# Splitting a decay step in two on VectorE, and a new order for the first two units, in a gated linear attention with two feed-forward layers

## What is computed

```python
B, H, S, D = 4, 8, 768, 48
state = zeros((B, H, D, D))
for t in range(S):
    state = alpha[:, :, t, :, None] * state + einsum('bhd,bhe->bhde', k[:, :, t], v[:, :, t])
    y[:, :, t] = einsum('bhd,bhde->bhe', q[:, :, t], state)
x = y.transpose(0, 2, 1, 3).reshape(3072, 384)
h = x @ w_in                                    # 384 -> 2048
x = (maximum(h, 0) + slope * minimum(h, 0)) @ w_out
h = x @ w_in2
g = where(h >= 1, h, where(h <= -1, 0, (h + 1) ** 2 / 4))
out = g @ w_out2
```

## Time and profile before

| | |
|---|---|
| median of 3 runs | 930.47 us |
| the profiled execution | 930.54 us, of which the span from first to last instruction is 928.8 us |
| TensorE busy | 906.5 us (98%) |
| VectorE, ScalarE, GpSimd busy | 449.1, 300.7, 293.2 us |
| mean granted TensorE clock | 0.996 of full |

### The profile page before, as it was taken

One profiled execution on the slowest core, in us unless ns is written; L12 is line 12 of the kernel. 1 busy time (PEld: TensorE's weight loads), 2 busy tenths in 40 slices (PEclk: granted clock), 3 DMA queues, 4 the chain that ended last, 5 costly groups with the idle time before them and its releaser, 6 DMA issues.

```text
span 928.8 us, 14324 instructions
## 1 busy us (share of the span) xinstructions
PE 906.5 (98%) x5774; PEld 761.3 (82%) x5774; DVE 449.1 (48%) x614; ACT 300.7 (32%) x561; POOL 293.2 (32%) x267
## 2 busy tenths in 40 slices
PE   8989989999999999999999999999999999999997
PEld 8888978887887888788888888888888888888886
DVE  6886755555655655555335543333333333333332
ACT  3532323223232332332245443233332332332322
POOL 3422212222222222222234334334343243243232
PEclk9999999999999999999999999999999999999999
DMA  8421211211111111110113200000100100100101
GB/s 283 153 68 50 75 42 39 66 40 40 49 40 39 39 40 41 45 60 1 68 35 97 74 1 1 20 14 1 35 1 1 35 0 1 35 1 1 34 1 35
DMA packets 31986, 39.47 MB, mean 42 GB/s; under 512 B 2096, under 2 KB 25136, under 8 KB 31920
## 3 DMA queue, kind: packets, MB, share of 16 engines
q1 hardware_dynamic: 31920, 38.55, 13.8%
HBM read 33.82 MB, written 4.72 MB: 41 GB/s over the span
## 4 chain that ended last, share of the span: by engine, by line
issue 66%; POOL 30%; PE 3%; ACT 0%; POOLq 0%; ACTq 0%
POOL g_lo L342 27%; POOL x_lo L349 2%; PE h_ps L712 1%; POOL p_last L336 0%; POOLq L174 0%; PE y_ps L717 0%; ACT w_hi L383 0%; PE y_ps L719 0%; PE y_ps L718 0%; PE y_ps L658 0%; PE a_ps L658 0%; PE y_ps L680 0%; PE a_ps L680 0%; PE h_ps L717 0%; ACT g L422 0%
## 5 line engine op out<-in xcount | busy, mean ns | idle before, releaser
L342 POOL TENSOR_TENSOR g_lo<-g,g_hi 128x512 fp32r<-128x512 f32 (+1 forms) x208 | 255.2, 1227 | 588.2 <-ACT g_hi L429 588.1
L422 ACT ACTIVATE g<-h_ps 128x512 f32<-128x512 f32 (+1 forms) x208 | 117.6, 565 | 503.5 <-PE h_ps L719 500.6
L717 PE MATMUL h_ps<-x_lo,w_hi 128*128 128x512 f32 (+1 forms) x624 | 240.8, 386 | 11.8 <-DVE x_lo L556 10.1
L717 PE MATMUL y_ps<-g_lo,w_hi 128*128 128x512 f32 (+1 forms) x624 | 233.7, 374 | 1.6 <-POOL g_lo L342 1.4
L719 PE MATMUL h_ps<-x_hi,w_lo 128*128 128x512 f32 (+1 forms) x624 | 233.9, 375 | 0.0
L718 PE MATMUL h_ps<-x_hi,w_hi 128*128 128x512 f32 (+1 forms) x624 | 233.6, 374 | 0.0
L719 PE MATMUL y_ps<-g_hi,w_lo 128*128 128x512 f32 (+1 forms) x624 | 233.0, 373 | 0.0
L718 PE MATMUL y_ps<-g_hi,w_hi 128*128 128x512 f32 (+1 forms) x624 | 232.9, 373 | 0.0
L569 DVE SCALAR_TENSOR_TENSOR g<-g 128x512 f32<-128x512 f32 x96 | 66.5, 692 | 247.0 <-ACT g L422 247.0
L717 PEld LDWEIGHTS h_ps<-x_lo,w_hi 128*128 128x128 f32 x624 | 117.6, 188 | 36.7 <-DVE x_lo L556 11.8
L717 PEld LDWEIGHTS y_ps<-g_lo,w_hi 128*128 128x128 f32 x624 | 118.0, 189 | 23.8 <-POOL g_lo L342 1.7
(11 more groups left out here) (69 smaller groups left out, 484.9 us busy)
## 6 DMA issues: line engine op xcount, KB each, us to landing
qk_sb<-qk SPq DMA_DIRECT2D x24, 448.0 KB, 4.1
y_all<-w SPq DMA_DIRECT2D x16, 384.0 KB, 7.8
alpha_sb<-decays SPq DMA_DIRECT2D x24, 224.0 KB, 3.1
v_sb<-v SPq DMA_DIRECT2D x24, 192.0 KB, 4.0
y<-y_all SPq DMA_DIRECT2D x18, 256.0 KB, 2.6
qk_sb<-w SPq DMA_DIRECT2D x8, 384.0 KB, 3.2
alpha_sb<-w SPq DMA_DIRECT2D x4, 384.0 KB, 3.1
att<-w SPq DMA_DIRECT2D x4, 384.0 KB, 3.0
```

Of the source, the lines that this page charges most:

```text
L342: nc.gpsimd.tensor_tensor(g_lo[:, s % G_RING, 0:w_], g32[:, s % G32_RING, 0:w_], g_hi[:, s % G_RING, 0:w_].bitcast(F32), ALU.subtract).the ...
L422: nc.scalar.activation(g32[:, s % G32_RING, 0:w_], h_ps[s % 2][:, 0:w_], ACT.Relu, scale=-1.0 if first else 0.5, bias=0.0 if first else 0. ...
L717: nc.tensor.matmul(out_, wh, lo, start=start, stop=False)
```

## The change

The decay becomes two stages. `scan_decays(u)` (the two scans and the reciprocal) stands four steps ahead of the turn, so in the step in which unit u - 1 is turned, behind its `x_lo` and behind that step's activation. `scale_qk(u)` (the two multiplications) stands three steps ahead, before that step's activation. For units 0 and 1 the order changes on four engines, unit 1 gets buffers of its own for the token copies of k and of the outputs (in `inv` and `prod`), the outputs of a fresh unit are made head parity by head parity so that they can begin after the first mask, and the identity products are 20 at first and 3 in between.

```diff
-        for _stage, _lag in (("decay", 5), ("scores", 2), ("mix", 1), ("turn", 0)):
+        for _stage, _lag in (("scan", 4), ("scale", 3), ("scores", 2), ("mix", 1), ("turn", 0)):
-ORDER = ("turn", "scores", "mix", "decay")
-FIRST_PLAN = [("scores", 0), ("scores", 1), ("mix", 0), ("turn", 0), ("mix", 1), ("turn", 1)]
-WARM = 24
-FILL = {("scores", 0): 12, ("scores", 1): 1, ("mix", 0): 1, ("turn", 0): 1, ("mix", 1): 2, ("turn", 1): 2}
+ORDER = ("turn", "scores", "mix", "scale", "scan")
+WARM = 20
+FILL = 3
...
+        def k_tok_of(u):
+            return by_pair(inv[:, 0:PAIRS * ROWS]) if u == 1 else k_tok[:]
+
+        def o_tok_of(u):
+            return prod[:, 0:D_MODEL] if u == 1 else o_tok[:].rearrange("p h d -> p (h d)")
...
             copy_k(0)
             split_w(0)
             split_w(1)
+            copy_k(1)
+            split_w(2)
             copy_outputs(0)
-            copy_k(1)
+            copy_outputs(1)
             turn_hi(0)
-            copy_outputs(1)
-            split_w(2)
             turn_hi(1)
...
+            def scale_qk(u):
+                q, k = (qk_of(u)[0:ROWS, x] for x in range(2))
+                dve.wait_ge(qk_loaded[u % 2], 16 * load_count(u))
                 dve.wait_ge(inv_done, u + 1)
-                dve.wait_ge(qk_loaded[u % 2], 16 * load_count(u))
...
             mask(0)
             mask(1)
-            update_state(0)
             turn_lo(0)
             turn_lo(1)
+            update_state(0)
             update_state(1)
...
                         if stage == "mix":
                             update_state(u)
+                        if stage == "scale":
+                            scale_qk(u)
                     activate(s + AHEAD)
                     for stage, u in plan_of(s):
-                        if stage == "decay":
-                            decay(u)
+                        if stage == "scan":
+                            scan_decays(u)
...
             pe.wait_ge(ident_set, 2)
             idle_matmuls(WARM)
-            for stage, u in FIRST_PLAN:
-                attention(stage, u)
-                idle_matmuls(FILL.get((stage, u), 0))
+            scores(0)
+            idle_matmuls(FILL)
+            scores(1)
+            outputs(0)
+            outputs(1)
+            turn_outputs(0)
+            turn_outputs(1)
+            sum_state(0)
+            sum_state(1)
```

More of the change, by code:

```diff
@@ L388, in copy_k @@
                 act.wait_ge(k_turned, states_before(u) + 1)
-                ge(act, state_summed, states_before(u))
-                nc.scalar.activation(k_tok[:], turn_bank(u)[:, 0:PAIRS * P].rearrange("p (h r) -> p h r", h=PAIRS)[:, :, 0:ROWS],
+                ge(act, state_summed, states_before(u) if u >= 2 else 0)
+                nc.scalar.activation(k_tok_of(u), turn_bank(u)[:, 0:PAIRS * P].rearrange("p (h r) -> p h r", h=PAIRS)[:, :, 0:ROWS],
                                      ACT.Copy).then_inc(k_tok_done, 1)
@@ L394, in copy_outputs @@
                 act.wait_ge(outputs_done, u + 1)
-                ge(act, o_turned, u)
-                nc.scalar.activation(o_tok[:].rearrange("p h d -> p (h d)"), scores_bank(u, 0)[:, 0:D_MODEL],
+                ge(act, o_turned, u if u >= 2 else 0)
+                if u == 1:
+                    act.wait_ge(last_kept, 2)
+                nc.scalar.activation(o_tok_of(u), scores_bank(u, 0)[:, 0:D_MODEL],
                                      ACT.Copy).then_inc(o_tok_done, 1)
@@ L496, in split_w, with scan_decays @@
                                         ALU.subtract).then_inc(w_lo_done, 1)
-            def decay(u):
+            def scan_decays(u):
                 al = alpha_sb[0:ROWS, u % 2]
@@ L503, in decay @@
                 ge(dve, last_kept, u)
+                if u == 2:
+                    dve.wait_ge(o_turned, 2)
+                    dve.wait_ge(state_summed, 2)
                 nc.vector.tensor_tensor_scan(prod[0:ROWS], al[:, 0:SCAN], starts[0:ROWS], 0.0,
@@ L512, in decay @@
                                              ALU.mult, ALU.add).then_inc(inv_done, 1)
+            def scale_qk(u):
+                q, k = (qk_of(u)[0:ROWS, x] for x in range(2))
+                dve.wait_ge(qk_loaded[u % 2], 16 * load_count(u))
                 dve.wait_ge(inv_done, u + 1)
-                dve.wait_ge(qk_loaded[u % 2], 16 * load_count(u))
-                k = qk_of(u)[0:ROWS, 1]
                 nc.vector.tensor_tensor(k, k, by_pair(inv[0:ROWS])[:, :, 1:SEG], ALU.mult).then_inc(k_scaled, 1)
-                q = qk_of(u)[0:ROWS, 0]
                 nc.vector.tensor_tensor(q, q, by_pair(prod[0:ROWS])[:, :, 1:SEG], ALU.mult).then_inc(q_scaled, 1)
@@ L597, in _ @@
             dve.wait_ge(pads_set, 2)
-            decay(0)
-            decay(1)
+            for u in range(2):
+                scan_decays(u)
+                scale_qk(u)
             dve.wait_ge(causal_set, 2)
@@ L661, in scores, with outputs @@
                             last.then_inc(scores_done, 1)
-            def mix(u):
-                q, vs, o, sums = qk_of(u)[0:ROWS, 0], v_of(u), scores_bank(u, 0), scores_bank(u, 1)
+            def outputs(u):
+                q, vs, o = qk_of(u)[0:ROWS, 0], v_of(u), scores_bank(u, 0)
                 pe.wait_ge(v_loaded[u % 2], 16 * load_count(u))
+                halves = [slice(HALF * i, HALF * (i + 1)) for i in range(2)]
+                if fresh(u):
+                    for e in range(2):
+                        pe.wait_ge(masked, 2 * u + e + 1)
+                        for h in range(PAIRS):
+                            c = slice((2 * h + e) * HD, (2 * h + e + 1) * HD)
+                            for t in halves:
+                                last = nc.tensor.matmul(o[t, c], att_of(u)[:, e, h, t], vs[:, c], start=True, stop=True)
+                    last.then_inc(outputs_done, 1)
+                    return
                 for e in range(2):
                     pe.wait_ge(masked, 2 * u + e + 1)
-                if not fresh(u):
-                    pe.wait_ge(state_done, 2 * states_before(u - 1))
-                halves = [slice(HALF * i, HALF * (i + 1)) for i in range(2)]
+                pe.wait_ge(state_done, 2 * states_before(u - 1))
                 for h in range(PAIRS):
[L673 to L676, removed]
+                    for t in halves:
+                        nc.tensor.matmul(o[t, 2 * HD * h:2 * HD * (h + 1)], q[:, h, t], state[0:ROWS, u % 2, h],
+                                         start=True, stop=False)
                     for e in range(2):
@@ L679, in mix, with sum_state @@
                         for t in halves:
-                            last = nc.tensor.matmul(o[t, c], att_of(u)[:, e, h, t], vs[:, c], start=fresh(u),
-                                                    stop=fresh(u) or e == 1)
+                            last = nc.tensor.matmul(o[t, c], att_of(u)[:, e, h, t], vs[:, c], start=False, stop=e == 1)
                 last.then_inc(outputs_done, 1)
[L683 to L689, removed]
+            def sum_state(u):
+                if not keeps_state(u):
+                    return
+                vs, sums = v_of(u), scores_bank(u, 1)
+                pe.wait_ge(k_tok_done, states_before(u) + 1)
+                for h in range(PAIRS):
+                    for e in range(2):
+                        r, c = slice(ODD * e, ODD * e + HD), slice((2 * h + e) * HD, (2 * h + e + 1) * HD)
+                        last = nc.tensor.matmul(sums[r, c], k_tok_of(u)[:, h, r], vs[:, c], start=True, stop=True)
+                last.then_inc(state_summed, 1)
             def turn_outputs(u):
@@ L696, in turn_outputs @@
                     pe.wait_ge(x_lo_done, u)
-                o = o_tok[:].rearrange("p h d -> p (h d)")
                 for m in range(KT):
-                    last = nc.tensor.transpose(turn_bank(u)[:, m * P:(m + 1) * P], o[:, m * P:(m + 1) * P], ident[:])
+                    last = nc.tensor.transpose(turn_bank(u)[:, m * P:(m + 1) * P], o_tok_of(u)[:, m * P:(m + 1) * P], ident[:])
                 last.then_inc(o_turned, 1)
[L702 to L708, removed]
             def idle_matmuls(count):
@@ L764, in _ @@
                 for stage, u in plan_of(s):
-                    attention(stage, u)
+                    if stage == "turn":
+                        turn_outputs(u)
+                    if stage == "scores":
+                        scores(u)
+                    if stage == "mix":
+                        outputs(u)
+                        sum_state(u)
                 if s + AHEAD < STEPS:
```

## The result

The changed kernel takes 954.25 us (median of 4 runs, 950.16 to 957.01) against 930.55 us for the kernel before (median of 4): the ratio is 1.0257 (95% interval 1.0238 to 1.0277). The forecast was slower, 946.0 us in a range of 931 to 953. The sign and the places are right, the size is not: 23.7 us instead of 15.5. The runs also scatter more than the four of before, 6.9 us against 0.8, and the scatter follows the granted clock: 957.01 us at 0.982, 956.04 at 0.983, 952.45 at 0.987, 950.16 at 0.990. Over the 13 runs beside the first experiments the kernel before spreads over 3.6 us too, by its clock: 927.3 us at 0.998, 930.8 at 0.993.

The account below looks back on a forecast made before the run. TensorE was taken as the bound, busy 906.5 of 928.8 us. Terms 14.2 (512-wide) + 3.0 (256-wide) + 1.7 (clock) - 3.4 (start) = +15.5 us on 930.54 us: 946.0 us, range 931 to 953.

Parts of the forecast that it names:

- 512-wide steps, +14.2 us: Scores of units 9 to 23: q ready later, new TensorE waits of 1.15 or 1.54 us, less three block-end stalls: +14.2 us.
- The bound by whole exclusion: 512-wide steps: VectorE and GpSimd never overlap, `g_lo` keeps its full 1.28 us, q 0.2 us later: 3 us over 15 units.
- 256-wide steps, +3.0 us: Scores of units 2 to 8: later k delays turns, removed block-end stalls give some back: +3.0 us, bounds 0 to +6.
- The start, -3.4 us: Units 0 and 1: scores(1) start sooner, first product at 18.6 us instead of 22.24: -3.4 us, bounds -2.5 to -3.9.
- Clock, +1.7 us: Half clock follows one of the new waits of units 2 and 3, none of the 2.0 us ones: +1.7 us.
- Rival C: Half clock also follows the 2.0 us waits (+6.8 us) and both of units 2 and 3: 954.5 us; chance 0.08.
- Rival B: Scans behind the activation escape the extra time beside `g_lo`, 1.05 us (512) and 0.55 (256) per unit: 922.5 us; chance 0.12.
- Rival D: The start gains nothing, since weights or masks take the place of the wait removed: 949.4 us; chance 0.04.
- rival A: 512-wide steps: VectorE scales q at once, not overtaken by GpSimd; -0.1 us instead of 14.2: 931.7 us; chance 0.14.

Follow-up runs that it names:

- q first: The changed kernel with q scaled before k: 978.4 us (2 runs, 976.61 and 980.19).
- the kernel with filled waits: The changed kernel with idle identity products ahead of each unit's scores from unit 2 (8 in 256-wide steps, 4 in 512-wide): 943.8 us, ratio to before 1.0161.
- the stages alone: The kernel before with only the new place of scans and scales, its old start kept: 956.06 us.
- the whole decay four steps ahead: The changed kernel with the decay unsplit, behind the activation four steps before the turn, new start kept: 951.19 us, ratio 1.0239.
- the kernel filled in part: The changed kernel with 8 idle identity products ahead of the scores in the 256-wide steps only (units 2 to 8): 946.3 us.
- the new start alone: The kernel before with only the new start; the decay stays whole, five steps ahead of the turn: 926.65 us, ratio 0.9968.

## Why the prediction was right in kind and wrong in size

**512-wide steps, +14.2 us.** Right: from the turn of k of unit 8 to the end of the span the changed kernel takes 18.5 us more than the kernel before, and 4.5 of them are the three stretches of half clock there: 14.0 are left. The waits are 1.08 us with a turn of k (1.15 forecast) and 1.55 without (1.54), the block-end stalls of 1.54 us are gone, and `g_lo` sits between k and q. With q first the same 1.7 us fell on k, so it is GpSimd's turn, not the operand, that makes the second multiplication long. The bound by whole exclusion that the prediction took from the Trainium skill (SBUF — State Buffer, Who interferes with whom) would have given 0.2 us more a unit. This trace does not agree: the `g_lo` shown ends at 164.06, 1.13 us after the scaling of k ends at 162.93, where its own time is 1.28 us, and TensorE waits 1.08 us.

**256-wide steps, +3.0 us.** Right in kind, 1.0 us too high: with the waits filled in these steps alone, so without half clock, the way from the first product of step 2 to the turn of k of unit 8 takes 111.14 us, against 109.18 in the kernel before with its two stretches of half clock: 2.0 us more. The waits are 2.00 us for units 4 to 7 (2.0 forecast), 2.91 for units 2 and 3 (some 3.2), 1.28 for unit 8. From one turn of k to the next it is 15.19 us without half clock instead of 13.77, so 1.4 us where 1.5 was forecast, and 16.69 with it.

**The start, -3.4 us.** Right: the first product at 18.04 (18.6 forecast), that of step 2 at 21.89 (22.15), and 3.6 us as a change by itself.

**Clock, +1.7 us.** This is the step that failed. It read: "The four of about 2.0 us lie between 1.54 (none in three) and 2.73 (both); they are nearer to 1.54: 0", and let one of units 2 and 3 be followed by half clock. In the profiled execution it was nine stretches: three for units 2 and 3, three behind the four 2.0 us waits, one behind 1.28 us and two behind 1.55. The forecast put half clock behind its 1.54 us waits and behind unit 8 at nothing, and gave unit 3 at most one stretch. At the measured 1.5 us each, nine are 13.5 us, 11.8 more than the 1.7 taken; less some 2 us by which the waits and the start came out below forecast, that is about the 10.0 us between the forecast and the 956.04 us of this execution. The rest of the sum held: without its clock term it gives 944.3 us, and the kernel with filled waits, with one stretch left, took 943.8.

Rival C had half clock behind all the 2.0 us waits, at 954.5 with a chance of 0.08. That it meets the median, 954.25, is in part luck: it reckoned six stretches at 1.7 us where nine at 1.5 came, and it took over the waits and the start, which are some 2 us too high.

The error was to rank the waits by length alone and to draw a boundary from five of them, all at the same place in a step. Counted over units 2 to 23 in the profiled executions of the changed kernel, the stages alone, the whole decay four steps ahead and, for the 512-wide steps, the kernel filled in part, half clock lay behind all 4 waits of 2.91 us, 11 of 14 of 2.00, 1 of 3 of 1.28, 7 of 16 of 1.55 and none of 44 of 1.08; with q first, behind 10 of 15 of 1.50. Stalls of 1.5 to 1.6 us for `x_lo`, ahead of a long row of products, had none, six times in the kernel before and the one with the new start alone. So what TensorE does around a wait may matter, which was not tested, but it is not all: the same wait of unit 4, 7 or 8, with the same TensorE work around it, had half clock behind it in one of two kernels and not in the other. What decides among them stays open.

Rival B (the scans run free behind the activation) is refuted: `prod` took 2.27 us in the 512-wide steps, as before. Rival D is refuted by the start alone, rival A by q's 1.77 us.

## To carry to other kernels

Before a producer is moved later to let something else pass, find its consumer's slack in the trace: here it was 3 us against a shift of 4.4. The cure was the other direction, the work split and its pieces moved earlier, which removed the same stall and kept the slack (907.5 us against 954.3). The whole decay six steps ahead was not run, so it is not shown that the split is needed for it. Price a new TensorE wait as its length and, as an estimate from the counts above, 1.5 us for half clock behind most waits of 2 us, behind about half of those of 1.3 to 1.55 us, and behind none of 1.1 us; that holds for this kernel, and another one needs its own counts. Take a scatter of runs that follows the granted clock as a sign of such waits. Idle products in the waits are a cheap test that separates the two prices.

## What the runs showed of the hardware that was not expected

Half clock (1.2 GHz) followed an idle time as short as 1.28 us (once in three), where in the kernel before 1.54 us was followed by none in three. Nine stretches of 3.41 us lay in one execution; the mean clock of 0.982 to 0.990 speaks for a different number in each run, and the runs spread over 6.9 us. It was counted in one of the four alone. A stretch costs 1.5 us.

Idle products of the identity, eight in each of the long waits and four in the short ones, left one stretch in place of nine: 12.0 us of span.

A GpSimd subtraction that starts during one VectorE multiplication is let in before the next one, though that one is already queued: the second takes 1.77 us in place of 0.69, in either order of the two, in all 15 units of the 512-wide steps of the changed kernel and of the one with q first.
